# Preparing q and k for an attention loop: first pair loaded head by head into both halves of the partitions, the later pairs' parts made by GpSimd, the units alternated

## The reference

```python
q_bits = (q @ proj > 0);  k_bits = (k @ proj > 0)        # 6 bits per row
mask = bucket(q_bits)[:, None] == bucket(k_bits)[None, :]
scores = where(mask, scale * q @ k.T, -1e9)
attn = exp(scores - rowmax) / (rowsum + 1e-9)
x = attn @ v
e = argmax(x @ w_gate + modality_bias);  h = relu(x @ w1[e]);  x = gate * (h @ w2[e])
g = max(x @ w_in, 0) + alpha * min(x @ w_in, 0);  out = g @ w_out
```

## Time and profile before

| | |
|---|---|
| median of 3 runs | 694.49 us (693.3 to 696.13) |
| the profiled execution: time, span | 696.09 us, 694.2 us |
| busy: PE, PEld, DVE, ACT, POOL | 98%, 87%, 67%, 51%, 33% of the span |
| mean granted TensorE clock | 0.995 |
| first exponential starts, last one starts | 14.0 us, 258.0 us |
| the chain that ended last | PE 86%, DVE 6%, ACT 4%, POOL 2% |

### The profile page before, as it was taken

How to read it: one execution, slowest core, us unless ns; L and a number is a source line. 1 busy time by engine, 2 the same in 40 slices (tenths; PEclk the granted TensorE clock), 3 DMA queues, 4 the chain that set the end, 5 groups by cost and what they waited for, 6 DMA issues and landing times.

```text
span 694.2 us, 12084 instructions
## 1 busy us (share of the span) xinstructions
PE 679.9 (98%) x3960; PEld 604.4 (87%) x3962; DVE 463.2 (67%) x975; ACT 356.6 (51%) x721; POOL 228.2 (33%) x311
## 2 busy tenths in 40 slices
PE   7799999999999999999999999999999999999998
PEld 4699999998989989889989998888888888888886
DVE  6688988989999988622511216666676666666664
ACT  5698988888788794124311215333343333433332
POOL 6865646565577871411013300600017000010000
PEclk9999999999999999999999999999999999999999
DMA  6965957657454420692112108200003000010001
GB/s 185 226 195 126 262 170 193 216 139 225 119 138 126 164 72 25 222 325 106 45 60 80 42 31 271 62 0 0 0 14 108 0 0 1 0 61 0 0 0 60
DMA packets 43872, 70.70 MB, mean 102 GB/s; under 512 B 4076, under 2 KB 21308, under 8 KB 43828
## 3 DMA queue, kind: packets, MB, share of 16 engines
q1 hardware_dynamic: 38548, 57.50, 28.9%
q0 software_dynamic: 2832, 8.45, 4.0%
q10 hardware_dynamic: 2448, 4.20, 1.6%
HBM read 33.59 MB, written 17.30 MB: 73 GB/s over the span
## 4 chain that ended last, share of the span: by engine, by line
PE 86%; DVE 6%; ACT 4%; POOL 2%; issue 1%; DMA 1%; ACTq 0%; DVEq 0%; POOLq 0%
PE bank L1215 6%; PE bank L1216 6%; PE bank L1217 6%; PE bank L990 6%; PE bank L1227 6%; PE bank L1228 6%; PE bank L1229 6%; PE bank L1007 4%; PE bank L1156 3%; PE bank L1158 3%; PE bank L1160 3%; PE bank L1009 3%; PE bank L973 3%; PE bank L1120 3%; PE bank L1119 3%; PE bank L1118 3%
## 5 line engine op out<-in xcount | busy, mean ns | idle before, releaser
L1331 ACT ACTIVATE probs<-bank,raffine 128x768 f32<-128x768 f32 x96 | 95.4, 994 | 30.2 <-DVE raffine L1624 29.5
L1616 DVE TENSOR_REDUCE bank<-bank 128x1 f32<-128x768 f32 x96 | 92.3, 961 | 9.4 <-PE bank L974 8.5
L990 PE MATMUL bank<-cst,probs 128*128 128x128 f32 x576 | 82.7, 275 | 2.5 <-DVE pt_lo L1632 1.6
L990 PEld LDWEIGHTS bank<-cst,probs 128*128 128x128 f32 x576 | 66.8, 140 | 13.4 <-issue 5.4
L1485 ACT ACTIVATE wi_hi<-ff_raw 128x512 fp32r (+1 forms) x48 | 30.4, 633 | 91.5 <-PE bank L1217 89.3
L1632 DVE TENSOR_TENSOR pt_lo<-bank,pt_hi 128x384 fp32r<-128x384 f32 x128 | 70.4, 551 | 8.7 <-ACT pt_hi L1348 7.6
L1007 PE MATMUL bank<-pt_hi,v_split 128*128 128x384 f32 x192 | 73.2, 381 | 3.1 <-POOL pt_lo L685 3.1
L1902 DVE SCALAR_TENSOR_TENSOR ht_lo<-bank,ht_hi 128x512 fp32r<-128x512 f32 x28 | 19.0, 689 | 85.2 <-ACT ht_hi L1427 85.2
L1215 PE MATMUL bank<-x_hi,wi_hi 128*128 128x512 f32 (+1 forms) x192 | 74.4, 387 | 0.0
L1216 PE MATMUL bank<-x_lo,wi_hi 128*128 128x512 f32 (+1 forms) x192 | 73.9, 385 | 0.0
L1217 PE MATMUL bank<-x_hi,wi_lo 128*128 128x512 f32 (+1 forms) x192 | 73.9, 385 | 0.0
(11 more groups left out here) (311 smaller groups left out, 1607.5 us busy)
## 6 DMA issues: line engine op xcount, KB each, us to landing
stacks<-nat SPq DMA_DIRECT2D x84, 192.0 KB, 4.0
y_slots<-zeros SPq DMA_DIRECT2D x14, 512.0 KB, 5.4
w_raw<-in_moe_w SPq DMA_DIRECT2D x6, 1024.0 KB, 9.9
ff_raw<-in_moe_w_in SPq DMA_DIRECT2D x8, 512.0 KB, 6.2
ff_raw<-in_moe_w_out SPq DMA_DIRECT2D x4, 1024.0 KB, 9.8
y_slots<-y_sb ACTq DMA_DIRECT2D x14, 256.0 KB
v_raw<-in_v SPq DMA_DIRECT2D x16, 192.0 KB, 3.6
x_rows<-x_out SPq DMA_DIRECT2D x8, 384.0 KB, 3.1
```

What stands on the lines that cost most here:

```text
L990: mm = pe.transpose(lane[1 + hf][:, t * P:t * P + P], probs[:, m % 3, kt * P:kt * P + P], C["ident"])
L1331: act.activation(probs[:, m % 3, :].rearrange("p (a c) -> p a c", a=2), s_ps[m % 2], ACT.Exp, bias=raffine[:, col, 1:2], scale=raffine[:, ...
L1616: dve.tensor_reduce(rmin_ps[n % 2], s_ps[n % 2], AX.XY, ALU.min).then_inc(rmin_done, 1)
```

## The change

- **First pair.** q and k of pair 0 are no longer loaded as a pair. Each head is loaded into both halves of the partitions (`q_twice`, `k_twice`), head 0 in halves of the columns, head 1 whole, right behind it without a wait. hi and lo are then written straight into `aq`, `bq`, `ak`, `bk`, without shifts and without DMAs. The features of pair 0 take two matmuls for each head and half (16 in all) in place of three for each half (12 in all); head 1's are units in steps 2 and 3, held in other banks. Two zeroed weight tiles `w_same`, `w_both` are added.
- **Later pairs.** From pair 2 on both parts of q and k are made by GpSimd in `parts_of`: for q a scaling in place, a copy and a subtraction, for k a copy and a subtraction. It waits for the load, for the previous pair's stacks and for its features. ScalarE and VectorE keep only pair 1's.
- **Order.** `UNIT` alternates: fq0, k0, fold, fq1, k1, fold, fk0, q0, fold, fk1, q1, fold.
- **SyncE.** First loads in another order, the gate's DMAs moved here from GpSimd (their layout made ahead in memory), `load_q` and `load_k` ahead of `stack_feats("fk")`.
- **GpSimd.** Ahead of the loop: two more zeroing instructions, lo of head 1's k, a copy of head 1's q, `split_v(0)`, the pair weights; the constants move to step 18, the first `split_v(1)` to step 5.

```diff
-WARM = (9, 12, 9, 3)
+WARM = (10, 1, 1, 4, 4)
-        UNIT = [("k", 0), ("k", 1), "fold", ("fq", 0), ("fq", 1), "fold",
-                ("fk", 0), ("fk", 1), "fold", ("q", 0), ("q", 1), "fold"]
+        UNIT = [("fq", 0), ("k", 0), "fold", ("fq", 1), ("k", 1), "fold",
+                ("fk", 0), ("q", 0), "fold", ("fk", 1), ("q", 1), "fold"]
-        EARLY_UNITS = [[], [("q", 0, 1), ("q", 1, 1)], [("k", 0, 1), ("k", 1, 1)],
-                       [("fq", 0, 1)], [("fq", 1, 1)], [("fk", 0, 1)], [("fk", 1, 1)], []]
+        EARLY_UNITS = [[], [], [("fk", 0, 0), ("fk", 1, 0)], [("fq", 0, 0), ("fq", 1, 0)], [], [("fq", 0, 1)],
+                       [("fq", 1, 1)], [("fk", 0, 1), ("q", 0, 2)], [("fold", 0, None)], [("fk", 1, 1)], [("q", 1, 2)],
+                       [("fold", 1, None)]]
...
+            sp.dma_start(k_twice[:, 0, 0:HALF], head_twice(k, 0, slice(0, HALF))).then_inc(k_first[0], 16)
+            sp.dma_start(q_twice[:, 0, 0:HALF], head_twice(q, 0, slice(0, HALF))).then_inc(q_first[0], 16)
             sp.dma_start(cst[:, 0:N_EARLY], consts[:, 0:N_EARLY]).then_inc(cst_in, 16)
-            for hf in range(2):
-                sp.wait_ge(q_first[hf], 16)
+            sp.dma_start(k_twice[:, 1], head_twice(k, 1, slice(0, SEQ))).then_inc(k_second, 16)
+            sp.dma_start(q_twice[:, 1], head_twice(q, 1, slice(0, SEQ))).then_inc(q_second, 16)
...
+            def parts_of(kind, hf, pair):
+                cols = slice(hf * HALF, hf * HALF + HALF)
+                if hf == 0:
+                    pool.wait_ge((q_in if kind == "q" else k_in)[pair % 2], 16 * ((pair + pair % 2) // 2))
+                    for hd in range(2):
+                        pool.wait_ge((q_stacked if kind == "q" else k_stacked)[hd], stacks(pair - 1))
+                hi, lo = halves(kind)
+                src = raw(kind, pair)[:, cols]
+                if kind == "q":
+                    pool.tensor_scalar(src, src, -SCALE, None, ALU.mult).then_inc(q_scaled, 1)
+                    pool.wait_ge(q_scaled, 2 * (pair - 2) + hf + 1)
+                pool.wait_ge(feat_made, feat_no("f" + kind, hf, pair - 1) + 1)
+                hi_done, lo_done = (q_hi_done, q_lo_done) if kind == "q" else (k_hi_done, k_lo_done)
+                pool.tensor_copy(hi[:, cols], src).then_inc(hi_done, 1)
+                pool.wait_ge(hi_done, split_no(hf, pair))
+                pool.tensor_tensor(lo[:, cols], src, hi[:, cols], ALU.subtract).then_inc(lo_done, 1)
...
+            pool.wait_ge(first_k_hi, 3)
+            pool.tensor_tensor(bk[BOT, 0, 1], k_twice[BOT, 1], ak[BOT, 0, 1], ALU.subtract).then_inc(b_on_pool, 1)
+            pool.wait_ge(first_q_hi, 3)
+            pool.tensor_copy(aq[BOT, 0, 1], bq[BOT, 0, 1]).then_inc(b_on_pool, 1)
+            pool.wait_ge(b_on_pool, 2)
             split_v(0)
...
                 if 0 <= n - 2 < STEPS and on_pool(n - 2, 1):
                     turned(n - 2)
-                for kind, hf, pair in units_at(n) if n >= len(EARLY_UNITS) else ():
-                    if kind == "k":
-                        k_lows(hf, pair)
+                for kind, hf, pair in units_at(n):
+                    if kind in ("q", "k"):
+                        parts_of(kind, hf, pair)
...
+            def first_q_low(hf):
+                cols = slice(hf * HALF, hf * HALF + HALF)
+                dve.wait_ge(first_q_hi, hf + 1)
+                dve.scalar_tensor_tensor(aq[BOT, 0, 0, cols], q_twice[BOT, 0, cols], -SCALE, bq[BOT, 0, 0, cols],
+                                         ALU.mult, ALU.subtract).then_inc(first_q_lo, 1)
...
+            for kind, hf in (("fk", 0), ("fk", 1), ("fq", 0)):
+                first_features(kind, hf, 0, first_bank(kind, hf))
+            first_q_low(1)
...
+                if n == 1:
+                    first_features("fq", 1, 0, first_bank("fq", 1))
+                    dve.wait_ge(first_q_hi, 3)
+                    dve.scalar_tensor_tensor(aq[TOP, 0, 1], q_twice[TOP, 1], -SCALE, bq[TOP, 0, 1],
+                                             ALU.mult, ALU.subtract).then_inc(first_q_lo, 1)
```

More of the change, by code:

```diff
@@ L384, in build, with halves, stacks, bit_columns @@
         TOP, BOT = slice(0, HD), slice(HD, P)
[L386 to L395, removed]
+        def halves(kind):
+            return (nat[:, 0], nat[:, 1]) if kind == "q" else (nat[:, 2], nat[:, 3])
+        def stacks(pair):
+            return 16 * STACK_PARTS * pair
+        def bit_columns(tile, rows=slice(None)):
+            return tile[rows].rearrange("p s (g c) -> p s g c", g=2)[:, :, :, 0:FEATS]
+        def pair_columns(tile, rows):
+            return tile[rows, :, HD:HD + FEATS] if rows == TOP else tile[rows, :, 0:FEATS]
         def raw(kind, pair):
@@ L442, in stack_q @@
                     sp.wait_ge(score_made, 2 * QT * (pair - 1))
[L443 to L448, removed]
+                q_hi, q_lo = halves("q")
+                for hd in range(2):
                     of, hi_to, lo_to = (TOP, TOP, BOT) if hd == 0 else (BOT, BOT, TOP)
@@ L459, in stack_k @@
                     sp.wait_ge(score_made, 2 * QT * (pair - 1))
[L460 to L465, removed]
+                k_hi, k_lo = halves("k")
+                for hd in range(2):
                     of = TOP if hd == 0 else BOT
@@ L765, in _ @@
                     turned(n - 2)
-                for kind, hf, pair in units_at(n) if n >= len(EARLY_UNITS) else ():
-                    if kind == "k":
-                        k_lows(hf, pair)
-                if n % QT == QT - 1 and 2 <= (n + 1) // QT < BH:
+                if n == HT:
+                    for hf in range(2):
+                        k_lows(hf, 1)
+                for kind, hf, pair in units_at(n):
+                    if kind in ("q", "k"):
+                        parts_of(kind, hf, pair)
+                if n % QT == QT - 1 and (n + 1) // QT < BH:
                     split_v((n + 1) // QT)
+                if n == 3 * QT:
+                    constants()
                 if n % QT == 1 and 0 <= n // QT - 2 < BH - 1:
@@ L881, in _, with first_feats @@
         def _(pe):
+            def first_feats(kind, hf, hd, p_ps):
+                side = kind == "fq"
+                cols = slice(hf * HALF, hf * HALF + HALF)
+                k_rows, q_rows = (TOP, BOT) if hd == 0 else (BOT, TOP)
+                twice, low, rows = (bq, aq, q_rows) if side else (ak, bk, k_rows)
+                no = 3 if hd else hf + 1
+                pe.wait_ge(w_made, 2)
+                pe.wait_ge(w_low_made, 1)
+                pe.wait_ge(first_q_hi if side else first_k_hi, no)
+                pe.matmul(p_ps, w_both[:, int(side)], twice[:, 0, hd, cols], start=True, stop=False)
+                if side:
+                    pe.wait_ge(first_q_lo, no)
+                elif hd:
+                    pe.wait_ge(b_on_pool, 1)
+                else:
+                    pe.wait_ge(a_k_lo, no)
+                pe.matmul(p_ps, w_same[rows, int(side)], low[rows, 0, hd, cols], start=False, stop=True
+                          ).then_inc(feat_made, 1)
             def feats(kind, hf, pair, p_ps):
-                hi, lo = halves(kind[1], pair)
+                hi, lo = halves(kind[1])
                 side, made, split = (1, q_hi_done, q_lo_done) if kind == "fq" else (0, k_hi_done, k_lo_done)
                 cols = slice(hf * HALF, hf * HALF + HALF)
+                pe.wait_ge(pair_w_made, 4)
                 pe.wait_ge(made, split_no(hf, pair))
@@ L1402, in _ @@
                     turned(n - 2, 1)
+                if n in (1, 3):
+                    for hf in range(2):
+                        high(("q" if n == 1 else "k", hf, 1))
                 for unit in units_at(n):
-                    high(unit)
+                    if unit[0] == "rows":
+                        high(unit)
                 for fc in PIECES.get(n, ()):
@@ L1778, in step @@
                     for unit in units:
-                        low(unit)
+                        if unit[0] not in ("q", "k"):
+                            low(unit)
+                if n in (4, 5):
+                    low(("q", n - 4, 1))
                 if 56 <= n < STEPS + 2:
```

311 lines of the change are left out of this document (151 added, 160 removed).

## The result

| | before | after |
|---|---|---|
| median | 694.38 us (693.3 to 696.13, 4 runs) | 728.99 us (727.55 to 729.4, 4 runs) |
| ratio | | 1.0492, 95% interval 1.0466 to 1.0518 |
| profiled execution: time, span | 696.09, 694.2 us | 729.03, 726.9 us |
| mean granted TensorE clock | 0.995 | 0.969 |
| first exponential starts | 14.0 us | 39.21 us |

The account below looks back on a forecast made before the run. The attention loop was taken as nearly TensorE's own time, with gains only in the start, early holes and hidden waits. -4.0 - 4.0 + 4.3 = -3.7 on 696.1 gave 692.4, as a median 690.8 us; range 683.5 to 697.5.

Parts of the forecast that it names:

- The first arrival: Start of the kernel: first loads are as large as before, so their arrival was taken as unchanged.
- part 1: The start up to step 12: gain of 4.0 us, bounds 1 and 6.5.
- The first low parts: Start: VectorE's second q low or GpSimd's head 1 subtraction holds the other; first minimum at 10.5 us, between 9.6 and 11.8.
- The rival of the shared port: Start: VectorE's low part held through GpSimd's early chain, minimum at 14.4, step 12 gain about 0, time 694.8 us; chance 15%.
- VectorE's pace to step 8: Start: VectorE sets the pace with 20.8 us of work; minimum of step 8 at 31.3 in place of 35.85.
- Part 2: Steps 12 to 72: alternation and less ScalarE and VectorE work take back waits; gain 4.0 us, bounds 1 and 6.4.
- Part 3: Steps 72 to 84: second chunk's load lands later, behind k's stack, delaying `values(76)`; loss 4.3 us, bounds 0 and 5.5.
- The scaling on GpSimd: GpSimd's q parts from pair 2 on: the scaling taken at 0.5 us, at most 1.01.
- the slower rival: Each pair's first step: k features land too late, 1.2 us in each of 7 pairs, time 699.2 us; chance 10%.
- The chunk's wait: Around step 81: rival that the wait for the second chunk is absorbed, time 686.5 us; chance 27%.
- the hole at step 81: Sign for the forecast: one TensorE hole of about 4 us behind GpSimd's 8 to 9 us wait for the second chunk.
- step 12 after 42.5: Sign against the forecast: the prediction is wrong if step 12 starts after 42.5 us.

Follow-up runs that it names:

- two_dmas: The changed kernel with each doubled load (one DMA for both partition halves) issued as two DMAs of 64 partitions: 699.5 us, ratio 1.0062 to before.
- outer2: The changed kernel with doubled loads still one DMA of leading dimension 2, but reading two different pairs instead of repeating one: 728.72 us (1 run).
- both: The changed kernel with each doubled load as two DMAs and load_chunk(1) issued ahead of stack_k(7): 693.75 us, ratio 0.9976 to before.
- spread: Kernel both with head 1's four feature units one in each of steps 1 to 4, not two each in steps 2 and 3: 691.79 us.
- alt_only: The kernel before with only UNIT alternated (early units of pairs 1 and 2 fitted to it): 698.87 us, ratio 1.0047.
- old_order: Kernel both with UNIT from step 12 on in the order of before, GpSimd still making the parts: 696.37 us, ratio 1.0005 to before.
- chunk_first: The changed kernel with load_chunk(1) issued ahead of stack_k(7) instead of behind it: 721.67 us, ratio 1.0386 to before.
- spread_chunk2: Kernel spread with the third chunk's load moved to right behind the k stack: 691.89 us, ratio 0.9947 to before.
- late_q: Kernel spread_chunk2 with GpSimd's parts of pair 2's q in steps 10 and 12 instead of 7 and 10: 690.43 us, ratio 0.9929 to before.

## Why the prediction was wrong

I forecast 690.8 us and a range up to 697.5; it is 728.99. One sentence of the forecast fails and carries most of the error; of the other mechanisms several were there, at other prices.

- **The first arrival (part 1), the step that failed:** "Loads are as large as before, so I leave the first arrival alone." The first four loads are as large (192 KB each), but their shape is another, and pair 0 as a whole now writes 1536 KB in place of 768. The new source has a leading dimension of 2, and with such DMAs in the queue the share fell to 0.13, about two engines of sixteen (2/16 = 0.125), and the rate to 48 GB/s; the DMAs behind them waited too. Cost: 29.5 us (two_dmas against after); outer2 shows that it hangs on the leading dimension of 2 and not on the repeated reading. The Trainium skill's page "DMA: Bandwidth & Descriptors", section "Rules for kernel authors", states it: an outermost dimension smaller than 16, a leading broadcast of c copies for example, confines the whole DMA to at most c engines. The traces agree (0.13). At the measured 48 GB/s one half of k (192 KB) takes 4.1 us, against 1.1 at the 174 of the earlier trace rows, and all six doubled loads take 33 us; the last of them landed at 38.4. I had none of this among the rivals, and no rival reached above 699.2.
- **The first low parts (part 1):** the number came out, in part by luck. I expected the minimum at 10.5, between 9.6 and 11.8, by whether VectorE's second q low or GpSimd's subtraction comes first. In both it came at 10.69, but neither of the two held it: VectorE's k lows ended at 6.92 and not at 6.1, GpSimd's subtraction began at 9.96 and not at 8.3, the second q low took 0.56 us, and the minimum waited 0.66 us for the scores. In two_dmas the subtraction came first (from 9.84, 1.81 us) and the q low beside it took 1.24 us, but the minimum, at 13.38 and so 1.6 later than I allowed, again waited for TensorE, whose scores began late, at 11.50, and ran slowly:

```profile
11.50 0.88 PE L1018 MATMUL bank<-stacks 128*128 128x384 f32 x1
...
13.38 0.97 DVE L1655 TENSOR_REDUCE bank<-bank 128x1 f32<-128x768 f32 x1 [1.32 <-PE bank L1019]
```

  The same matmul takes 0.41 us in both. The rival of the shared port gave 14.4, but what it describes, VectorE held through GpSimd's whole chain, didn't happen. Why TensorE was slow there is open: the granted clock in that window (10 to 13) is 1.00.
- **VectorE's pace to step 8 (part 1):** right in size once the units are spread (I gave 31.3 for the minimum of step 8; it is 30.60 in spread), wrong for the kernel as it was changed (35.34 in both, 35.85 before). I summed VectorE's work and didn't ask who waits for each piece. Two feature units in one step make TensorE wait for the compare between them; step 12 came at 44.03 in both in place of about 40.7, and the gain of 4.0 was 0.65 there. spread gets the rest back up to step 12, and pays 2.0 us of it in steps 12 to 24.
- **Part 2:** 4.0 us forecast for steps 12 to 72. Before takes 152.63, alt_only 148.96 (-3.7), both 150.02 (-2.6), after 151.20 (-1.4), old_order 152.31 (-0.3). The size is right for the alternation, the reason half wrong, since I put two things together that don't add. In steps 24 to 48 only the alternation acts: old_order gains 0.20 us on before, both and alt_only 1.06. From step 48 to 72 each of the two gains alone (alt_only 2.10, old_order 1.76) and together they gain less (1.04). That this is VectorE's routing work meeting a busier GpSimd, as I wrote, is argued and not tested.
- **Part 3:** the event is right to 0.3 us: I put the chunk's arrival at 219.25 and the release of `values` at 225.8, and in two_dmas, where step 72 is 0.5 us earlier than before's, they are at 218.96 and 225.64. The price was not: 4.3 forecast, 5.75 (two_dmas against both) to 7.3 (after against chunk_first) measured. What the sum left out is TensorE's restart at the low clock: 8.68 - 2.69 - 4.70 = 1.3 us in two_dmas, and in after 1.3 in step 81 and 1.7 more in step 82. Why steps 72 to 84 of chunk_first are still 1.2 us longer than before's 30.29 is only partly explained, by the third chunk's 0.8.
- **The scaling on GpSimd:** taken at 0.5 us, bounds 0.50 and 1.01; it took 1.17. In the steady pairs it cost nothing (59.14 us for steps 24 to 48 in both and in alt_only), as GpSimd had the room (23.68 of 30 us in the window 60 to 90).
- **Rivals:** in the changed kernel no pair's first step waited for k's features, so the slower rival didn't happen there. Its event does show in two variants, once each, at pair 7's first step (step 84): 1.03 us in spread and 1.73 in old_order (at step 12 the waits are 0.21 to 0.31 us, in spread, spread_chunk2 and late_q). The chunk's wait was not absorbed. Of the signs that I named, the hole at step 81 came, and so did the one against me, step 12 after 42.5 (71.17).
- **The bounds:** those of the three parts add up to -12.9 and +3.5, and not to -12 and +4. That changes nothing: the loss of the start was in none of them.

The sum with the measured terms, against the profiled execution's 696.1: start to step 12 +26.5, steps 12 to 72 -1.4, 72 to 84 +7.9, 84 to 95 -0.3, together +32.7 and 728.8; the execution took 729.03.

## What to carry to other kernels

Before taking a transfer as unchanged because its bytes are, compare its pattern: which dimension stands in front, and how long it is. When all engines idle and the DMA share is low too, look for the transfer everybody waits for and for issues that hold the queue. Price a hole on TensorE higher than the wait itself: here 4.70 us of waiting cost 6.0. And when work is moved to balance engines, change the order first: here the order of the units gave all the gain of the steady pairs (1.06 us of 60.20 in steps 24 to 48), and each move of work brought a new place where something else stood in line behind a wait.

## What the runs showed of the hardware

- DMAs with a leading dimension of 2 (step 0 in after, a real step in outer2) ran at a share of 0.13 to 0.14 and 48 GB/s and held up those behind them: issues of 3.90, 7.88 and 9.38 us, where the two-DMA form has 0.43 to 0.65 for each, and 65 KB of constants, issued at 2.13, took 16.5 us to land (3.7 before, 4.1 in two_dmas). The row is from the DMA issues of after: size, us from issue to landing.

```profile
cst<-in_consts SPq DMA_DIRECT2D x1, 65.0 KB, 16.5
```

- TensorE came back from 4.70 us without work at a granted clock of 0.56 over the next 3.4 us (two_dmas), and from 5.00 us at 0.50 over the next 6, although it was busy 5.96 of them (after).
- VectorE's low part of q over 64x384 took 0.56 us alone and 1.24 beside GpSimd's 1.81 us subtraction (two_dmas).
- GpSimd's multiplication by a constant in place, 128x384 float32, takes 1.17 us; the cast of the same tile takes 0.50 and the subtraction of two tiles 1.01. The profile of both, the durations of that line (min, median, max in ns):

```profile
L690 POOL TENSOR_SCALAR q_even<-q_even x6: 1166/1169/1179, 39.1 to 158.7; 128x384 f32<-128x384 f32 x6
```
